# Delta-rule stage: first merge with 64x64 operands, turned block made on VectorE, logits of four steps side by side, keys loaded first

## The reference

```python
k_n = k / (np.linalg.norm(k, axis=-1, keepdims=True) + 1e-06)
for t in range(S):
    kt, vt, bt = (k_n[:, :, t], v[:, :, t], beta[:, :, t, None])
    y[:, :, t] = np.einsum('bhd,bhde->bhe', q[:, :, t], state)
    v_old = np.einsum('bhde,bhd->bhe', state, kt)
    state = state + bt[:, :, :, None] * np.einsum('bhd,bhe->bhde', kt, vt - v_old)
...
logits = np.einsum('bsd,de->bse', x, w_gate)
local_gate = 1.0 / (1.0 + np.exp(-np.einsum('bsd,de->bse', x, w_local).squeeze(-1)))
```

## Time and profile before

| | us |
|---|---|
| median of 3 runs (570.93 to 577.87) | 572.61 |
| the profiled execution | 574.82 |
| its span, first to last instruction | 573.3 |
| of it the delta-rule stage, to the last copy of logits | 211.7 |
| TensorE busy over the span | 494.7 |
| VectorE busy over the span | 359.9 |

### The profile page before, as it was taken

The page is one execution under the profiler, slowest core; times in us unless marked ns, Lnnn a source line. Parts: engine busy times, 40 slices in busy tenths (PEclk is TensorE's granted clock), DMA queues, the critical chain, the costliest instruction groups (busy, mean ns, idle before and its releaser), DMA issues.

```text
span 573.3 us, 17109 instructions
## 1 busy us (share of the span) xinstructions
PE 494.7 (86%) x7104; PEld 456.8 (80%) x7104; DVE 359.9 (63%) x545; ACT 289.3 (50%) x469; POOL 88.6 (15%) x127
## 2 busy tenths in 40 slices
PE   5989798979899973008999999999998689999997
PEld 5778698878889962006989898989898579999997
DVE  3895459623110126606999999999994347689671
ACT  2514233222222334207998989999994135454533
POOL 2614132004000001840010101010100520000000
PEclk9988759575655695557999999999999779999999
DMA  9752011008000014436555764574100320000202
GB/s 140 129 97 45 19 31 31 5 3 278 18 3 5 3 36 187 180 138 233 174 187 196 268 234 158 172 259 137 55 14 29 109 70 1 0 2 1 83 1 83
DMA packets 60834, 54.66 MB, mean 95 GB/s; under 512 B 41155, under 2 KB 54339, under 8 KB 60774
## 3 DMA queue, kind: packets, MB, share of 16 engines
q1 hardware_dynamic: 53638, 40.98, 24.6%
q0 software_dynamic: 3968, 12.19, 6.2%
q10 hardware_dynamic: 3168, 0.59, 0.8%
HBM read 76.16 MB, written 12.19 MB: 154 GB/s over the span
## 4 chain that ended last, share of the span: by engine, by line
PE 49%; issue 2%; DVE 2%; DMA 1%; ACT 1%; POOL 0%; DVEq 0%; POOLq 0%; ACTq 0%
PE ps L1683 5%; PE ps L1685 4%; PE ps L1684 4%; PE ps L1700 4%; PE ps L1701 4%; PE ps L1702 4%; PE ps L1954 3%; PE ps L1955 3%; PE ps L1956 3%; PE ps L1967 3%; PE ps L1968 3%; PE ps L1969 3%; PE ps L1692 3%; PE ps L1673 1%; PE ps L1942 1%
## 5 line engine op out<-in xcount | busy, mean ns | idle before, releaser
L1641 DVE TENSOR_TENSOR w2l<-raw,w2h 128x768 fp32r<-128x768 f32 x76 | 67.7, 953 | 6.7 <-ACT w2h L1584 6.7
L1641 DVE TENSOR_TENSOR w1l<-raw,w1h 128x1024 fp32r<-128x1024 f32 x54 | 62.9, 1220 | 3.3 <-ACT w1h L1584 1.2
L1584 ACT CAST w2h<-raw 128x768 fp32r<-128x768 f32 x76 | 58.3, 854 | 0.6 <-DMA raw<-in_moe_w_dram 0.6
L1700 PE MATMUL ps<-w2h,hh 128*128 128x384 f32 x152 | 52.4, 344 | 1.8 <-DVE hl L1646 1.8
L1584 ACT CAST w1h<-raw 128x1024 fp32r<-128x1024 f32 x54 | 53.3, 1065 | 0.7 <-DMA raw<-in_moe_w_dram 0.7
L1702 PE MATMUL ps<-w2h,hl 128*128 128x384 f32 x152 | 50.9, 335 | 0.0
L1701 PE MATMUL ps<-w2l,hh 128*128 128x384 f32 x152 | 50.8, 334 | 0.0
L1683 PE MATMUL ps<-w1h,xh 128*128 128x512 f32 x114 | 47.4, 416 | 1.6 <-DVE xl L1633 1.6
L1685 PE MATMUL ps<-w1h,xl 128*128 128x512 f32 x114 | 45.7, 401 | 0.0
L1684 PE MATMUL ps<-w1l,xh 128*128 128x512 f32 x114 | 45.3, 398 | 0.0
L1954 PE MATMUL ps<-mh,wih 128*128 128x384 f32 x96 | 34.0, 354 | 1.3 <-DVE ml L1879 1.3
(11 more groups left out here) (215 smaller groups left out, 1150.9 us busy)
## 6 DMA issues: line engine op xcount, KB each, us to landing
raw<-in_moe_w_dram SPq DMA_DIRECT2D x57, 512.0 KB
raw<-in_moe_w_dram SPq DMA_DIRECT2D x76, 384.0 KB
x_sorted<-x_all SPq DMA_DIRECT2D x1, 3648.0 KB, 13.3
x_all<-x_sorted POOLq DMA_DIRECT2D x19, 192.0 KB, 2.8
y_sorted<-x_all POOLq DMA_DIRECT2D x19, 192.0 KB, 2.2
...
```

What stands on the lines that cost most here:

```text
L1584: act.copy(hi(par), raw).then_inc(s_wh, 1)
L1641: dve.tensor_tensor(lo(par), raw, hi(par).bitcast(F32), ALU.subtract).then_inc(s_wl, 1)
L1700: pe.matmul(psY[par], hh[:, i, c], w2h[:, par, f], start=(f == 0), stop=False)
```

## The change

Six parts.

1. **First merge.** The operands that stay in the array (Moff, IZ) become 64x64 block-diagonal, two for each unit in place of four 32x32 ones. `z16` and `merged` issue 32 matmuls each in place of 64. ScalarE's `off_blocks` and VectorE's `one_plus` write two halves each, so one operation more for each.
2. **Turned block.** `merged_t` and `xt_copy` go; VectorE's `x_turned(g)` turns X64's first half into XT.
3. **Logits.** `logits(p)` takes four steps at once: `wg`, padded to 32 columns, stays in the array, in four column blocks side by side, and the transposed outputs stream through. The result is turned back by one transpose (`logits_back`). 12 sets of 3 matmuls become 3 sets of 12 matmuls and a transpose.
4. **w_mul** writes PSUM bank 0 instead of `BW`, and no longer waits for the router's copies.
5. **Keys first.** The keys of four steps are loaded and transposed before the queries; `products` of the first four steps is split in `prod_m` (keys) and `prod_q` (queries), and the key masks run first. The lists of all engines are written anew.
6. `warm(n)` uses matmuls of up to 512 columns; `kq` becomes a ring of 9 steps.

```diff
+            load_k(0, (0,))
+            load_k(1, (0,))
+            load_q(0)
             load_v(0)
             load_k(2)
+            load_q(1)
+            load_k(3)
...
-                act.activation(Moff[:, g % 2, :, SB:BLK], Mf[:, g // GR % 2, g % GR * U:(g % GR + 1) * U, SB:BLK],
-                               ACT.Copy, scale=low16[:, 0:1]).then_inc(s_off, 1)
+                for i in range(2):
+                    act.activation(Moff[:, g % 2, :, i * BLK + SB:(i + 1) * BLK],
+                                   Mf[:, g // GR % 2, g % GR * U:(g % GR + 1) * U, SB:BLK],
+                                   ACT.Copy, scale=low16[:, i:i + 1]).then_inc(s_off, 1)
...
-                act.copy(w_sb[:, n % 2].rearrange("p h d -> p (h d)"), bank[BW][:, 0:H * D]).then_inc(s_w, 1)
+                act.copy(w_sb[:, n % 2].rearrange("p h d -> p (h d)"), bank[0][:, 0:H * D]).then_inc(s_w, 1)
...
+                act.copy(xTr[:, m % LB], bank[BW][:, 0:CD * P]).then_inc(s_rc, 1)
+            def logits_turned(p):
+                act.wait_ge(s_lp, p + 1)
+                act.copy(lgT[:], bank[BW][:, CD * P:CD * P + P]).then_inc(s_lt, 1)
+            def logits_copy(p):
+                act.wait_ge(s_ln, p + 1)
+                act.copy(lg[:, p * LB:(p + 1) * LB],
+                         bank[BW][:, CD * P:CD * P + P].rearrange("p (j e) -> p j e", j=LB)[:, :, 0:E + 1]).then_inc(s_lg, 1)
...
-                dve.tensor_tensor(IZ[:], blocks(BX), eye32[:].unsqueeze(1).to_broadcast([P, U, BLK]),
-                                  ALU.add).then_inc(s_iz, 1)
+                dve.wait_ge(s_cst, NCST)
+                if g:
+                    dve.wait_ge(s_xp, g)
+                for i, half in enumerate((first, second)):
+                    dve.scalar_tensor_tensor(out=IZ[:, :, i * BLK:(i + 1) * BLK], in0=blocks(BX), scalar=half[:, 0:1],
+                                             in1=eye32[:, i].unsqueeze(1).to_broadcast([P, U, BLK]),
+                                             op0=ALU.mult, op1=ALU.add).then_inc(s_iz, 1)
+            def x_turned(g):
+                dve.wait_ge(s_x0, g + 1)
+                if g:
+                    dve.wait_ge(s_z32, g)
+                dve.transpose(XT[:], X64[:, g % 2, :, 0, :]).then_inc(s_xtc, 1)
...
                 if other is not None:
                     pe.wait_ge(other, value)
-                for _ in range(count):
-                    o = pe.matmul(bank[i][:, 0:P], ident[:], ident[:], start=True, stop=True)
+                while count:
+                    w = min(count, NBLK)
+                    o = pe.matmul(bank[i][:, 0:w * P], ident[:], ident[:].unsqueeze(1).to_broadcast([P, w, P]),
+                                  start=True, stop=True)
+                    count -= w
                 o.then_inc(s_warm, 1)
...
+            def products(n, cols=slice(0, 2)):
                 pe.wait_ge(s_kc, n + 1)
-                pe.wait_ge(s_qc, n + 1)
-                if n < 2:
-                    pe.wait_ge(s_bc, 1)
-                elif n < EARLY:
-                    pe.wait_ge(s_gq, n - 1)
-                i = pair(n)
+                i, s, c0 = pair(n), n % NR, cols.start * STEP
+                w = (cols.stop - cols.start) * STEP
                 for m in range(NP):
                     for r in range(R):
                         for b in range(B):
-                            o = pe.matmul(bank[i + r][tok[b], m * P:(m + 1) * P], kq[row[r], n, 0, m, tok[b]],
-                                          kq[row[r], n, :, m, tok[b]], start=True, stop=True)
-                o.then_inc(s_gr, 1)
+                            o = pe.matmul(bank[i + r][tok[b], m * P + c0:m * P + c0 + w], kq[row[r], s, 0, m, tok[b]],
+                                          kq[row[r], s, cols, m, tok[b]], start=True, stop=True)
+                return o
+            def prod_m(n):
+                if n < 2:
+                    pe.wait_ge(s_bc, 1)
+                else:
+                    pe.wait_ge(s_gm, n - 1)
+                products(n, slice(0, 1)).then_inc(s_gr, 1)
+            def prod_q(n):
+                pe.wait_ge(s_qc, n + 1)
+                if n < 2:
+                    pe.wait_ge(s_gm, n + 3)
+                else:
+                    pe.wait_ge(s_gq, n - 1)
+                products(n, slice(1, 2)).then_inc(s_gp, 1)
+            def prod_both(n):
+                pe.wait_ge(s_qc, n + 1)
+                if n < EARLY:
+                    pe.wait_ge(s_gq, n - 1)
+                products(n).then_inc(s_gp, 1)
...
             def z16(g):
                 pe.wait_ge(s_dt, 2 * (g // GR) + 1)
-                pe.wait_ge(s_off, g + 1)
+                pe.wait_ge(s_off, 2 * (g + 1))
                 if g:
                     pe.wait_ge(s_x64, 2 * g)
                 for u in range(U):
-                    for i in range(NBLK):
-                        o = pe.matmul(blocks(BX)[quad[i], u], Moff[quad[i], g % 2, u],
-                                      DT[quad[i], g % GR * U + u], start=True, stop=True)
+                    for b in range(B):
+                        o = pe.matmul(blocks(BX)[tok[b], u], Moff[tok[b], g % 2, u], DT[tok[b], g % GR * U + u],
+                                      start=True, stop=True)
                 o.then_inc(s_z16, 1)
...
             def merged(g):
-                pe.wait_ge(s_iz, g + 1)
+                pe.wait_ge(s_iz, 2 * (g + 1))
                 pe.wait_ge(s_dt, 2 * (g // GR) + 2)
                 for u in range(U):
-                    for i in range(NBLK):
-                        o = pe.matmul(blocks(BX)[quad[i], u], IZ[quad[i], u], Dm[quad[i], g % GR * U + u],
+                    for b in range(B):
+                        o = pe.matmul(blocks(BX)[tok[b], u], IZ[tok[b], u], Dm[tok[b], g % GR * U + u],
                                       start=True, stop=True)
                 o.then_inc(s_xp, 1)
-            def merged_t(g):
+            def z32(g):
+                pe.wait_ge(s_xtc, g + 1)
                 pe.wait_ge(s_x0, g + 1)
                 pe.wait_ge(s_x1, g + 1)
-                for u in range(U):
-                    for b in range(B):
-                        i = 2 * b
-                        o = pe.matmul(blocks(BX)[quad[i], u], Dm[quad[i], g % GR * U + u], IZ[quad[i], u],
-                                      start=True, stop=True)
-                o.then_inc(s_xtp, 1)
-            def z32(g):
-                pe.wait_ge(s_xtc, g + 1)
                 for u in range(U):
                     for b in range(B):
...
-            def w_mul(n, left=None, value=0):
+            def w_mul(n):
                 g, st = divmod(n, GS)
                 pe.wait_ge(s_r, n + 1)
                 if st == 0:
                     pe.wait_ge(s_x64, 2 * (g + 1))
-                if left is not None:
-                    pe.wait_ge(left, value)
                 for h in range(H):
                     for b in range(B):
-                        o = pe.matmul(bank[BW][tok[b], h * D:(h + 1) * D],
+                        o = pe.matmul(bank[0][tok[b], h * D:(h + 1) * D],
                                       X64[tok[b], g % 2, st * H + h].rearrange("p c t -> p (c t)"),
                                       r_sb[tok[b], h], start=True, stop=True)
...
-            def logits(m, left=None, value=0):
-                pe.wait_ge(s_rc, m + 1)
-                if m == 0:
+            def logits(p, left=None, value=0):
+                pe.wait_ge(s_rc, LB * (p + 1))
+                if p == 0:
                     pe.wait_ge(s_wg, 32)
                 if left is not None:
                     pe.wait_ge(left, value)
                 for c in range(CD):
-                    o = pe.matmul(bank[BW][:, CD * P:CD * P + E + 1], xTr[:, m % 2, c * P:(c + 1) * P], wg[:, c],
-                                  start=(c == 0), stop=(c == CD - 1))
+                    for j in range(LB):
+                        o = pe.matmul(bank[BW][quad[j], CD * P:CD * P + P], wg[:, c],
+                                      xTr[:, j, c * P:(c + 1) * P], start=(c == 0), stop=(c == CD - 1))
                 o.then_inc(s_lp, 1)
+            def logits_back(p, left=None, value=0):
+                pe.wait_ge(s_lt, p + 1)
+                if left is not None:
+                    pe.wait_ge(left, value)
+                pe.transpose(bank[BW][:, CD * P:CD * P + P], lgT[:], ident[:]).then_inc(s_ln, 1)
```

544 lines of the change are left out of this document (268 added, 276 removed).

## The result

The changed kernel takes 551.4 us (median of four runs, 544.6 to 561.0) beside 572.9 us (570.9 to 577.9) of the kernel before, a ratio of 0.9539 with a 95% interval of 0.941 to 0.9668: faster.

A forecast was written before the change was run, and what follows sets the result against it. TensorE's instruction list, at its granted clock, was taken to set the pace. First w_mul at 50.9 us, work 172 x 0.72 = 124.1 and 9.6 idle gave 184.6, so -27.1: 547.7, taken as 548 us (535 to 559; all but extremes 524 to 570).

The forecast's parts named there:

- the 184.6 of the sum: End of the delta-rule stage: 50.9 us to the first w_mul, 124.1 of TensorE work and 9.6 idle; 27.1 us earlier.
- The first `w_mul`: Before the recurrence: keys first and the reordered lists start it at 50.9 us in place of 56.9, -6.0 us.
- The chain behind DT: From VectorE's turned result to the first w_mul: turns, norms, merges, copies and hand-overs one behind the other, 15.6 us.
- The clock: Stage after the first w_mul: h, the share of TensorE work at half clock, falls from 0.60 to 0.35.
- Half-clock stretches behind `w_mul(0)`: Sign to look for in the profile: TensorE's half-clock stretches together near 60 us.
- the prediction's argument against the wide form: Clock rose at 151.9 us amid merged's 128 quadrant records; the wide form streams half as much in its time.
- The idle time: TensorE after the first w_mul: 13.7 us, less 8 of stalls, plus 3 to 4 of new waits: 9 to 10.
- The new waits on VectorE: TensorE in the stage: waiting for VectorE adds 3 to 4 us of idle time.
- The work: TensorE's stage at half-clock prices: 170 us, merges +8.7, logits -11.7, transposes +2.4, fillers +2.6, gives 172.
- The rival in which column blocks do not overlap: Logits: each set costs four times as much, +14 us at half clock, about +10, 558 us; chance 0.05.
- the slower rival: Wide merges stream too little, the clock falls at z16(1) and stays at half: +16, 591 us; chance 0.04.
- as before: Rival for the stage: the clock behaves as before, 0.60 of work at half clock, 565 us (559 to 571); chance 0.25.

The follow-up runs named there:

- Experiment 4: Changed kernel with twelve more warming products ahead of prod_q(3), where TensorE had stood 2.2 us: 544.0 us, ratio 0.947 to the kernel before.
- experiment 7: Changed kernel with more warming products ahead of the first merge, and DT straight behind VectorE's substitution, ahead of the query masks: 547.8 us, ratio 0.946 to the kernel before.
- experiment 1: The changed kernel run again without any edit: 551.0 us, ratio 0.950 to the kernel before.
- experiment 9: Changed kernel with twelve more warming products, and SyncE's one 3.6 MB transfer of zeros cut into seven paced pieces: 544.3 us, ratio 0.944 to the kernel before.
- experiment 11: Changed kernel with five satisfied waits added ahead of each product of z16 and merged: 616.2 us, ratio 1.064 to the kernel before.
- experiment 2: Changed kernel with z16 and merged in 32x32 quadrants again, nothing else: 566.1 us, ratio 0.975 to the kernel before.
- 10: Changed kernel with quadrant merges, turned block on TensorE and 128-wide logits weights all taken back at once: 582.5 us, ratio 1.023 to the kernel before.
- experiment 8: Changed kernel with the four logits of each set written to one block of 32 columns, so nothing lies side by side: 551.1 us, one run.
- experiment 6: Changed kernel with twelve more warming products ahead of prod_q(3) and eight more at each of three later places: 551.3 us, ratio 0.970 to the kernel before.

## Why the prediction was right, and where it was wrong

The time was forecast at 548 and is 551.4, or 551.9 as the mean of ten runs. That it lies so near is partly luck. The two profiled executions of the changed kernel end their stage 13.8 and 12.2 us later than the 184.6 of the sum. Both were low draws of the clock (0.857 and 0.868 beside a mean of 0.878), and no profile shows a run near the median, so which terms made up the difference there is not known. Against the first profiled execution, whose stage ends at 198.4:

- **The first `w_mul`: -6.0 forecast, +1.1 measured, 7.1 us of the 13.8.** Two steps failed. The sum took z16(0) and what follows at full clock; TensorE stood 2.2 us ahead of prod_q(3), the clock went to half until 48.6 us, and z16(0) alone took 3.63 in place of 2.06. Experiment 4 covers the gap and has `w_mul(0)` at 53.1. And DT was placed at 35.3 and came at 36.84: VectorE's masks and folds made the turn start at 23.81 in place of 22.7, and the query masks took 2.6 us with their wait, not 2.1. The chain behind DT, summed at 15.6 us, held at full clock (53.12 - 37.32 = 15.8 in experiment 4) and took 21.2 here. With DT ahead of the masks it was 17.2 (experiment 7), for then VectorE's norms ahead of `x_turned`, which the chain left out, came last.
- **The clock: h of 0.35 forecast, 0.47 measured: 172.7 x 0.43 x 0.12 = 8.9 us.** In experiment 1 the same kernel had 0.33, so 0.35 was not a bad middle, and one profile could not have told. Half-clock stretches behind `w_mul(0)` were 83 us here where I said near 60, and 60 or so in experiment 1. What I had wrong is how much hangs on the stalls. Long pauses go with a fall: the one at 33 us does in eight profiles of eight, and the stall behind the transfer of zeros in four of five. But taking that stall away gained nothing by the medians (experiment 9), and the longest half-clock stretch of this profile, 110 to 178.3 us, has 1.4 us of idle time. What the kernels do show is that those with quadrants in all merges have h of 0.54 to 0.60, and those with wide merges 0.11 to 0.47 (experiment 11 aside). The reason is open, and the prediction's argument against the wide form, from the rise at 151.9 us, does not fit it.
- **The idle time: 9.6 forecast, 6.8 measured, 11.9 in experiment 1.** Right in kind and near in size: experiments 2 and 10, with quadrants, have 19 to 20. The new waits on VectorE (3 to 4 us) came to under 1 us here, 0.4 for the turned block and 0.2 for a mask.
- **The work: 172 forecast, 172.7 measured.** The prices held: 3.6 and 2.1 us for a merge (3.85 and 2.2), 1.5 for a set of logits (1.6), and `x_turned` 0.7 for 1.0. Term by term, taking back the merges is 13 less and the turn 9 more, so together the merges cost 4, not 8.7; the logits save 8, not 11.7. The two errors are of one size and cancel, which is luck.
- **The rival in which column blocks do not overlap** is refuted by experiment 8 (3.3 times). That the wide merges pull the clock down, the slower rival, is refuted by experiment 2, which is slower and more at half clock without them.
- **Two slips in the sum.** 172 x 0.7205 is 123.9 and not 124.1, which changes nothing. And the 0.75 for "faster" adds a third of "as before" in words and a sixth in numbers (559 to 561 of 559 to 571); with the third it would be 0.79.

Over all runs the mean clock is 0.852 before (44 runs of the experiments, mean 573.9 us) and 0.878 after (ten, 551.9). A line through the runs of either kernel, taken at 0.865, a clock that both had, gives 569 and 559: some 11 us of the 22 are there at the same clock, and some 11 are the clock itself. Of the first 11, idle time is 1.5 to 7 by the two profiles of the changed kernel (11.9 and 6.8 beside 13.4); the rest they don't place.

By its parts, by medians: the three edits inside the stage are worth 31 us together, the wide merges 15, the turned block 18 at most (4 of them from the place I gave it), the logits 3 to 4; the order around them, keys first and fillers, takes about 10 back, 3.4 of them that same uncovered copy. At equal clock they are smaller: 3.7, 9.5 and 3.4, beside 13.8 for all three at once. That a part which adds TensorE work is among the largest gains, I had seen as separate terms (work up, idle down, h down). Experiment 2 has the same terms: work and idle time cancel, and h is what is left.

**Open**: what lifts and drops the clock where there are no pauses (110 to 178 us in the first profile, at half clock with 1.4 us of idle time). Clumps of full-width products did not lift it for good (experiment 6). Why kernels with quadrants have the lower clock, and why the same program is given such different patterns, was not tried. Whether the count of instructions alone makes the stalls is open too, since experiment 11 put waits in place of products.
